# Attention in chunks: VectorE's scans first, its products together, GpSimd behind them, the state's decay on ScalarE

## What is computed

```python
for t in range(S):
    kt, vt, rt, wt = (k[:, :, t], v[:, :, t], r[:, :, t], w[:, :, t])
    cur = np.einsum('bhd,bhe->bhde', u[None] * kt, vt)
    y[:, :, t] = np.einsum('bhd,bhde->bhe', rt, state + cur)
    state = wt[:, :, :, None] * state + np.einsum('bhd,bhe->bhde', kt, vt)
```

## Time and profile before

| | us |
|---|---|
| median of 3 runs | 867.24 (866.93 to 870.03) |
| the profiled execution | 866.79 |
| its span, first to last instruction | 865.1 |

### The profile page before, as it was taken

The page is one execution under the profiler, slowest core; times in us unless marked ns, Lnnn a source line. Parts: engine busy times, 40 slices in busy tenths (PEclk is TensorE's granted clock), DMA queues, the critical chain, the costliest instruction groups (busy, mean ns, idle before and its releaser), DMA issues.

```text
span 865.1 us, 21623 instructions
## 1 busy us (share of the span) xinstructions
PE 756.5 (87%) x5663; PEld 666.0 (77%) x5664; DVE 537.1 (62%) x1409; ACT 394.5 (46%) x764; POOL 148.9 (17%) x177
## 2 busy tenths in 40 slices
PE   0687988989359999999999999839999999999994
PEld 0566776767348898988888888838999999989993
DVE  4999999999647557464657557445454363526621
ACT  1455656557316445363546446305444252525520
POOL 3332534435300000000000000000011001000100
PEclk9999989889769999999999999969999999999998
DMA  3554668643265334233335334133443342514110
GB/s 61 135 139 111 158 150 234 184 132 103 106 218 165 97 113 143 74 107 105 102 109 175 102 104 152 66 103 112 136 153 109 109 155 71 185 37 154 65 40 25
DMA packets 50270, 103.77 MB, mean 120 GB/s; under 512 B 7921, under 2 KB 29904, under 8 KB 50224
## 3 DMA queue, kind: packets, MB, share of 16 engines
q1 hardware_dynamic: 30080, 67.77, 26.2%
q10 hardware_dynamic: 15024, 21.17, 9.1%
q0 software_dynamic: 5120, 14.26, 4.6%
HBM read 85.73 MB, written 19.01 MB: 121 GB/s over the span
## 4 chain that ended last, share of the span: by engine, by line
PE 62%; DVE 23%; issue 5%; ACT 3%; SPq 2%; ACTq 2%; DMA 1%; DVEq 0%; another core or an unknown queue 0%; POOL 0%; POOLq 0%
PE bank L1242 17%; PE bank L1268 15%; PE bank L1276 9%; PE bank L1247 8%; PE bank L1257 5%; DVE SF L721 3%; DVE Q L708 3%; DVE Rq L716 3%; PE bank L1209 2%; PE bank L1231 2%; ACT wall L519 2%; DVE YT L756 2%; DVE dv L729 2%; DVE Kb L704 2%; DVE St L748 1%
## 5 line engine op out<-in xcount | busy, mean ns | idle before, releaser
L1242 PE MATMUL bank<-wall,xT_hi 128*128 (+1 forms) x660 | 180.8, 410 | 3.0 <-ACT xT_hi L607 3.0
L1268 PE MATMUL bank<-wall,hT_hi 128*128 x880 | 166.9, 341 | 0.7 <-ACT hT_hi L616 0.5
L1268 PEld LDWEIGHTS bank<-wall,hT_hi 128*128 128x128 f32 x880 | 154.4, 189 | 8.0 <-issue 5.6
L817 DVE TENSOR_TENSOR wall<-raw,wall 128x1024 f32 (+1 forms) x96 | 112.0, 1221 | 61.8 <-ACT wall L519 58.5
L1242 PEld LDWEIGHTS bank<-wall,xT_hi 128*128 128x128 f32 x660 | 119.9, 192 | 23.9 <-issue 2.6
L611 ACT ACTIVATE hs<-bank 128x512 f32<-128x512 f32 x110 | 65.1, 592 | 112.8 <-PE bank L1247 105.7
L519 ACT ACTIVATE wall<-raw 128x1024 f32 (+1 forms) x96 | 95.0, 1049 | 42.0 <-issue 42.0
L1247 PE MATMUL bank<-wall,xT_lo 128*128 (+1 forms) x330 | 95.5, 398 | 0.6 <-DVE xT_lo L976 0.6
L616 ACT ACTIVATE hT_hi<-bank 128x512 fp32r<-128x512 f32 x110 | 59.8, 597 | 77.4 <-PE bank L1257 77.4
L1276 PE MATMUL bank<-wall,hT_lo 128*128 x440 | 91.2, 348 | 0.0
L976 DVE TENSOR_TENSOR xT_lo<-bank,xT_hi 128x384 fp32r<-128x384 f32 x57 | 31.8, 558 | 84.6 <-ACT xT_hi L607 84.6
(11 more groups left out here) (192 smaller groups left out, 1024.3 us busy)
## 6 DMA issues: line engine op xcount, KB each, us to landing
raw<-wall_in SPq DMA_DIRECT2D x96, 512.0 KB, 3.8
xin<-sorted ACTq DMA_DIRECT2D x59, 194.0 KB
rk<-rk_in SPq DMA_DIRECT2D x48, 192.0 KB
wb<-w_in SPq DMA_DIRECT2D x48, 96.0 KB
v_in<-v_src ACTq DMA_DIRECT2D x24, 192.0 KB, 2.5
vT<-vT_in ACTq DMA_DIRECT2D x48, 96.0 KB, 2.6
sorted<-padrow SPq DMA_DIRECT2D x16, 194.0 KB, 2.2
sorted<-yrow,slot POOLq DMA_INDIRECT x28, 2.7
```

The costliest lines, as they stand in the source:

```text
L817: v.tensor_tensor(w_lo[:, slot, cols], raw[:, q], w_hi[:, slot, cols].bitcast(F32), ALU.subtract).then_inc(w_split, 1)
L1242: pe.matmul(bank[n][:, :], xT_hi[:, k, :], w[:, bass.ds(slot, 1), cols].rearrange("p o n -> p (o n)"), start=(k == 0 and w is w_hi), stop= ...
L1268: pe.matmul(bank[2][:, 0:DM], hT_hi[:, j, :], w[:, bass.ds(slot, 1), W2 + j * DM:W2 + (j + 1) * DM].rearrange("p o n -> p (o n)"), start=( ...
```

## The change

- DVE's `pre` runs all its scans and reciprocals first, then `Rq` over 128x512, then `Kb` over 128x512 in one instruction (before: two of 128x256). `k_ready` counts one a unit. The router's `norms1`/`choose1` and `place1` become `route`, which runs between the scans and the products.
- POOL's `products(u)` waits for `k_ready` of the same unit. POOL's `ahead` is 2.
- The decay of the state is no longer a DVE instruction but four ScalarE copies, one a pair, with the decay as a per-partition scale: `decay(u - 1)` stands in ACT's step u behind `copy_row(u - 1)`. Its last copy increments `s_ready`. At the head of `pre(u)`, u > 2, DVE now waits for `s_ready` to reach min(u - 2, 20).
- The last chunk's increment, addition, decay and transposed keys are left out: nobody reads that state.

```diff
             def reload(u, c, b):
-                sp.wait_ge(k_ready, 2 * u + 2)
+                sp.wait_ge(k_ready, u + 1)
@@ gpsimd
             def products(u, b):
                 gp.wait_ge(rkw_in[b % 2], 64 * (b // 2 + 1) + 32 * (u - b))
+                gp.wait_ge(k_ready, u + 1)
@@
             def first(u, b):
-                products(0, 0)
-                products(1, 1)
+                products(u, b)
                 masks(u, b)
             def step(c, u, b, nu, nb):
                 if nu is not None:
-                    masks(nu, nb)
-                if u + 2 < UNITS:
-                    products(u + 2, (b + 2) % B)
+                    products(nu, nb)
...
+                if nu is not None:
+                    masks(nu, nb)
-            each_unit(gp, 1, first, step)
+            each_unit(gp, 2, first, step)
@@ scalar
+            def decay(u, b):
+                act.wait_ge(s_added, u + 1)
+                for a in range(PAIRS):
+                    last = act.activation(St[:, b, a, 0:D], St[:, b, a, 0:D], ACT.Copy, scale=Q[:, u % LIVE, a * C1 + C:a * C1 + C1])
+                last.then_inc(s_ready, 1)
@@
                 if u > 0:
                     copy_row(u - 1, (u - 1) // B, (b - 1) % B)
+                    if u <= UNITS - B:
+                        decay(u - 1, (b - 1) % B)
@@ vector
-            def pre(u, b):
+            def pre(u, b, route):
                 par, k = b % 2, u % LIVE
                 v.wait_ge(rkw_in[par], 64 * (b // 2 + 1) + 32 * (u - b))
+                if u > 2:
+                    v.wait_ge(s_ready, min(u - 2, UNITS - B))
@@
                     v.reciprocal(bank[7][:, LASTQ + C - 1:LASTQ + HSEG - 1:C1], whole[:, 2 * hf:2 * hf + 2, C]).then_inc(iq_ready, 1)
-                    if hf == 0:
-                        v.tensor_tensor(Rq[:, k], rk[:, par, 0], whole[:, :, 0:C], ALU.mult).then_inc(r_ready, 1)
-                    else:
-                        weigh(0)
                     v.wait_ge(iq_ready, 2 * u + hf + 1)
...
-                weigh(1)
+                route()
+                v.tensor_tensor(Rq[:, k], rk[:, par, 0], whole[:, :, 0:C], ALU.mult).then_inc(r_ready, 1)
+                v.tensor_tensor(Kb[:, k], rk[:, par, 1], SF.rearrange("p (a t) -> p a t", t=C1)[:, :, 0:C], ALU.mult).then_inc(k_ready, 1)
@@
-                v.wait_ge(su_done, u + 1)
-                v.tensor_tensor(St[:, b, :, 0:D], St[:, b, :, 0:D], bank[5]..., ALU.add).then_inc(s_added, 1)
-                v.wait_ge(s_added, u + 1)
-                v.tensor_tensor(St[:, b, :, 0:D], St[:, b, :, 0:D], bcast_inner(Q[...][:, :, C], D), ALU.mult).then_inc(s_ready, 1)
+                if c < NCHUNK - 1:
+                    v.wait_ge(su_done, u + 1)
+                    v.tensor_tensor(St[:, b, :, 0:D], St[:, b, :, 0:D], bank[5]..., ALU.add).then_inc(s_added, 1)
@@
-                v.wait_ge(s_ready, u + 1)
                 v.tensor_tensor(YT[:, c % 2, b], bank[6]..., dv[:, par], ALU.add).then_inc(yt_ready, 1)
@@ tensor
+                if c > 0:
+                    pe.wait_ge(s_ready, u - B + 1)
                 for a in range(PAIRS):
                     for q in halves:
                         pe.matmul(bank[6][q, a * C:(a + 1) * C], St[q, b, a, :], Rq[q, k, a, :],
```

More of the change, by code:

```diff
@@ L523, in step @@
                     copy_a(nu, nb)
-                    copy_kt(nu, nb)
+                    if nu < UNITS - B:
+                        copy_kt(nu, nb)
                 if c > 0 and b == 1:
@@ L696, in _ @@
             v.tensor_tensor(en[:, 8:9], en[:, 7:8], tau[:, 1:2], ALU.mult).then_inc(e_ready, 1)
-            def pre(u, b):
+            def pre(u, b, route):
                 par, k = b % 2, u % LIVE
                 v.wait_ge(rkw_in[par], 64 * (b // 2 + 1) + 32 * (u - b))
-                def weigh(hf):
-                    v.tensor_tensor(Kb[:, k, 2 * hf:2 * hf + 2], rk[:, par, 1, 2 * hf:2 * hf + 2],
-                                    SF[:, hf * HSEG:(hf + 1) * HSEG].rearrange("p (a t) -> p a t", t=C1)[:, :, 0:C], ALU.mult).then_inc(k_ready, 1)
+                if u > 2:
+                    v.wait_ge(s_ready, min(u - 2, UNITS - B))
                 for hf in range(2):
@@ L732, in step, with route @@
                 par = b % 2
+                def route():
+                    if c > 0 and b == 2:
+                        norms1(c - 1, c - 1)
+                        choose1(c - 1)
+                    if c > 0 and b == 3:
+                        place1(c - 1, c - 1, (c - 1) % 2)
                 if u == 0:
                     spread(0, 0, 0)
-                if c > 0 and b == 2:
-                    norms1(c - 1, c - 1)
-                    choose1(c - 1)
                 if nu is not None:
-                    pre(nu, nb)
+                    pre(nu, nb, route)
+                else:
+                    route()
                 if u + 1 < UNITS:
                     spread(u + 1, (u + 1) // B, (b + 1) % B)
-                if c > 0 and b == 3:
-                    place1(c - 1, c - 1, (c - 1) % 2)
-                v.wait_ge(su_done, u + 1)
-                v.tensor_tensor(St[:, b, :, 0:D], St[:, b, :, 0:D], bank[5][:, 0:PAIRS * D].rearrange("p (a e) -> p a e", a=PAIRS), ALU.add).then_inc(s_added, 1)
-                v.wait_ge(s_added, u + 1)
-                v.tensor_tensor(St[:, b, :, 0:D], St[:, b, :, 0:D], bcast_inner(Q[:, u % LIVE].rearrange("p (a t) -> p a t", t=C1)[:, :, C], D), ALU.mult)\
-                 .then_inc(s_ready, 1)
+                if c < NCHUNK - 1:
+                    v.wait_ge(su_done, u + 1)
+                    v.tensor_tensor(St[:, b, :, 0:D], St[:, b, :, 0:D], bank[5][:, 0:PAIRS * D].rearrange("p (a e) -> p a e", a=PAIRS), ALU.add).then_inc(s_added, 1)
                 if c > 1 and b == 0:
@@ L853, in _ @@
             link(v.tensor_copy(oh5[:, 0, 0], accbase[:, :]))
-            each_unit(v, 2, pre, step)
+            each_unit(v, 2, lambda u, b: pre(u, b, lambda: None), step)
             split_lo(0, 0, 0)
@@ L1052, in attend @@
                 k = u % LIVE
-                pe.wait_ge(k_ready, 2 * u + 2)
+                pe.wait_ge(k_ready, u + 1)
                 if u > 0:
@@ L1084, in back @@
                 pe.wait_ge(yt_ready, u + 1)
-                pe.wait_ge(kt_copied, min(u + 3, UNITS))
-                if u >= UNITS - 2:
+                pe.wait_ge(kt_copied, min(u + 3, UNITS - B))
+                if u >= UNITS - B - 2:
                     pe.wait_ge(sq_done, u)
@@ L1122, in step @@
                     diagonal(nu, nb)
-                    keys(nu)
+                    if nu < UNITS - B:
+                        keys(nu)
                 if u > 0:
                     pe.wait_ge(yt_ready, u)
+                if c > 0:
+                    pe.wait_ge(s_ready, u - B + 1)
                 for a in range(PAIRS):
@@ L1130, in step @@
                                   start=(a == 0), stop=False, skip_group_check=True)
-                pe.wait_ge(kt_copied, u + 1)
                 pe.wait_ge(v_loaded[b], 48 * (c + 1))
[L1134 to L1141, removed]
+                if c < NCHUNK - 1:
+                    pe.wait_ge(kt_copied, u + 1)
+                    if u > 0:
+                        pe.wait_ge(s_added, u)
+                    for a in range(PAIRS):
+                        for hf, q in enumerate(halves):
+                            h = 2 * a + hf
+                            last = pe.matmul(bank[5][q, a * D:(a + 1) * D], KT[:, par, a, q],
+                                             v_in[:, b, h * D:(h + 1) * D], start=True, stop=True, skip_group_check=True)
+                    last.then_inc(su_done, 1)
                 if c > 0 and b == 1:
```

## The result

| | before | after |
|---|---|---|
| median, us | 867.09 (866.38 to 870.03, 4 runs) | 1007.06 (1003.84 to 1010.07, 4 runs) |
| the profiled execution | 866.79 | 1003.84 |
| its span | 865.1 | 1002.1 |
| Kb of unit 2 to Kb of unit 22 | 162.7 | 303.2 |

The ratio is 1.161, with a 95% interval of 1.159 to 1.164. The prediction was 1018, with a range of 980 to 1040.

The account below looks back on a forecast made before the run. DVE was taken to bound the attention. Twenty cycles of 14.78 us (295.6) plus 17.6 for the router make 313.2 against 162.7 before; with the start 151.1 more on 866.8, so 1018 us, range 980 to 1040.

Parts of the forecast that it names:

- The hold: At pre's head: DVE waits for decay(u-1) behind copy_row, loses its lead; one chain PE, ACT, DVE, 14.78 us, 20 cycles.
- The cold step: Attend's start to copy_row's end with TensorE's clock low at first: 9.37 us, the middle of 8.96 and 9.78; warm 7.08.
- The four copies: The decay on ACT between copy_row and pre: 0.295 us each, 0.2 from start to start, 0.90 us in all.
- pre: DVE's scans, reciprocals, Rq and Kb in the new order: 4.38 us, then a 0.05 us hop to PE.
- The router: Its small DVE instructions now lie on the chain: 4.4 us in each of four chunks, 17.6 us.
- the low end: Lower edge of the cold-step case, with an 8.96 us step and the cheap copies: 1003 us.
- the rival's cycle: The 20 cycles if TensorE's clock stays high: 7.08 us replaces 9.37, diagonal waits 0.3 for rkp, 12.77 us each; chance 0.08.
- The start: SP's reload(0) waits for rkp(0) behind Kb(0): unit 2's data 1.4 us later, 0.6 left after pre(2)'s gain.
- The rival in which it stays high: TensorE's clock stays high all or most of the time through the 20 cycles: 976 us, chance 0.08.
- The regrouping: DVE's and POOL's new order: merging Kb's halves and moving the products brings about nothing; the 1.0 us Rq stall goes.
- DVE's floor of 5.8 us a unit: DVE's own work per attention unit, without the Rq stall and the decay: from 7.2 to about 5.8 us.
- The rival of 833 us: Faster: the s_ready wait is met anyway, units fall from 7.2 to PE's 5.9 us, about 833 us; chance 0.04.

Follow-up runs that it names:

- three routes: Changed kernel with four Q buffers 847.75 us; with the decay back on DVE 852.34 us; with the decay at the head of ACT's step 850.51 us.
- The hold alone: Kernel before plus only the four ScalarE decay copies behind copy_row and the waits on s_ready: 986.40 us, ratio 1.138.
- the added products: Changed kernel with 28 unread matrix products (42 at b = 2) behind back in PE's steps 1 to 20: 976.24 us, ratio 1.129 to the kernel before.
- the best kernel: Changed kernel with four Q buffers, decay at the head of ACT's step and POOL's wait for k_ready removed: 843.25 us, ratio 0.976 to the kernel before.

## Why the prediction was right, step by step

**The hold.** Right in place and mechanism: 20 waits, each released by the copies, the chain PE, ACT, DVE as written. Taking the hold away by three routes gave 848, 852 and 851 us. The hold alone gave 14 per cent.

**Where the 20 cycles differ.** 313.2 us were predicted, 303.2 measured. By terms:

- *The cold step*, attend's start to copy_row's end. This is the term that was mis-sized. It was 9.37 us, with 0.3 more at b = 1, 188.6 us for 20; the 20 in the trace add up to 175.3, 13.3 us less. The first of them (39.44 to 46.61, 7.17 us) was warm, since no long wait lay ahead of it. The others lie between 7.67 and 9.98 around a mean of 8.85. I took the middle of the first and the last of four cold steps at the routers, and these were not a fair sample. In those four (8.96, 9.33, 9.55 and 9.78 us) the granted clock was back at 1.0 at 4.6, 5.5, 5.9 and 6.4 us after attend's start, 5.6 on average; in the 19 cold steps of the changed kernel it was back at 3.0 to 6.2 us, 4.2 on average. The shorter stretch at the low clock fits the shorter step; what sets the moment of its return no run here isolates.
- *The four copies*: 0.90 predicted with 0.08 for the gaps, 1.00 measured from copy_row's end to the scans (105.64 to 106.64). One copy is 0.328 us long, not 0.295. ACT, changed kernel, 40 to 342 us:

```profile
L507 ACT ACTIVATE St<-St,Q 128x48 f32<-128x48 f32 x80 | 20.0, 328 | 0.0
```

  The estimate from the Trainium skill ("ScalarE: Activation LUTs", What ACT_TABLE_LOAD costs), 186 + 93 + 0.833 x 48 = 319 ns for one and 93 of overlap, was nearer than the one from lT, and the trace agrees with it: 328 ns for one, and 1.00 us for four.
- *pre*: 4.43 with the hop to PE predicted, 4.52 measured; 1.8 us in 20.
- *The router*: 2.4 + 0.7 at b = 2 predicted, 3.4 measured (the cycle from 111.16 to 129.27 is 18.11 us, less 9.21 for the step and 5.52 for copies and pre); 1.0 at b = 3, as predicted. 1.1 us in all.

13.3 less, and 0.4, 1.8 and 1.1 more, are the 10 us. Two small sums of the prediction were off without effect on this: the low end with 8.96 and the cheap copies is 1002, not 1003, and the rival's cycle is 12.79, not 12.77.

**The ends.** The start cost 0.4 us (0.6 predicted). From attend of unit 22 to the last YT's end is 16.1 us against 18.5, a gain of 2.4 where nothing was taken. I had written that the state work left out in the last chunk is hidden; it is not. Left out alone it gave 2 us, and with the hold it makes the difference between 18.5 and 16.0. Behind the last YT, where nothing was changed, the profiled execution was 1.6 us shorter than the one before. With the 10 us of the turns this makes up the 14 us between 1018 and the profiled 1003.84; the median is 3 us above that.

**The clock.** It fell in each of the 20 waits, as forecast, and its mean was 0.74 where I wrote 0.7. The rival in which it stays high was priced at 976 us, and with PE kept busy the kernel took 976.24. Its cycle was right, 12.8 us against 12.7 in the turns that the added products do not delay, but that the totals agree to a microsecond is luck: with those delays the 20 cycles took 275.5 us instead of 271, and from attend of unit 22 to the last YT's end it was 14.1 us against 18.5 before, where the price had no difference. The rule of the Trainium skill by which, for modelling, a ramp costs below 1% of a typical kernel's span ("TensorE: Matmul & The Clock Gate", What's actually happening) does not hold here: about 30 us of 1007, 3 per cent, since the low clock is paid for in 20 steps.

**The regrouping.** I said that merging Kb and moving the products brings about nothing, and counted the router as lying on the chain. The second is borne out: the router's place alone is 15 to 18 us. The first is not quite: on the chain the new order is 0.23 us a turn slower (4.52 against 4.29), 4.6 us in 20. DVE's floor of 5.8 us a unit was not reached in any run: with the hold gone, ordinary units mostly took 6.1 to 7.1 us, as PE waits for rkp and DVE for data. The rival of 833 us was 10 us too low even for the best kernel.

## What to carry to other kernels

Before moving an instruction to another engine's queue, write down what stands ahead of it there and what each of those waits for. If the moved instruction releases a buffer that the engine working ahead needs, its place in the queue sets how far ahead that engine can run, and a microsecond on the closed chain is paid in every turn. A buffer more, or the instruction a few lines earlier, was worth 154 to 159 us here. Work that stands between two dependent steps of such a chain is better placed ahead of the wait; here that took 15 to 18 us off.

## What the runs showed of the hardware that I had not expected

- The time from attend's start to the clock's return is not one number: in the changed kernel it was 3.0 to 6.2 us from turn to turn. In cycles of 13 to 18 us the step behind the wait took 7.7 to 10.0 us. Lengthening the cycle by 0.9 us added another 0.4 on average, half of it in PE's part.
- Filling PE's wait with matrix products that nobody reads made a kernel 3 per cent faster: the granted clock went from a mean of 0.74 to 1.00 over the stage.
- POOL's product moved out of the way of one DVE instruction fell on the next with two SBUF inputs: St times Q went from 0.36 to 0.75 us.
